# Two-branch attention with a routed mixture of experts on one core: the order of copies, scores and weighted sums within a head pair, and the engine of expert 0's low halves

## What is computed

```python
# attention, for each batch and head: the sum of two branches
q_d, k_d, v_d = means over 4 neighbouring tokens          # 144 rows
out_d = softmax(scale * q_d @ k_d.T) @ v_d                # downsampled branch
out_up = repeat(out_d, 4)
scores = where(|i - j| < 4, scale * q @ k.T, -1e9)        # local branch
x = out_up + softmax(scores) @ v                          # 2304 tokens x 512
# dense layer
h = x @ w_in; x2 = (h * cos(h)) @ w_out                   # 512 -> 2048 -> 512
# experts: each token goes to the one of 8 with the largest logit
e = argmax(x2 @ w_gate); g = softmax(x2 @ w_gate)[e]
out = g * (relu(x2 @ w1[e]) @ w2[e])                      # 512 -> 1024 -> 512
```

## Time and profile before

| | us |
|---|---|
| median of 3 executions | 1009.35 |
| lowest and highest | 1007.31 and 1009.55 |
| the profiled execution | 1010.8 |
| its span | 1009.1 |
| TensorE busy in it | 879.5 (87%) |
| VectorE busy | 563.1 (56%) |
| ScalarE busy | 388.0 (38%) |
| GpSimd busy | 340.0 (34%) |

### The profile page before, as it was taken

How to read it: one execution, slowest core, us unless ns; L and a number is a source line. 1 busy time by engine, 2 the same in 40 slices (tenths; PEclk the granted TensorE clock), 3 DMA queues, 4 the chain that set the end, 5 groups by cost and what they waited for, 6 DMA issues and landing times.

```text
span 1009.1 us, 16491 instructions
## 1 busy us (share of the span) xinstructions
PE 879.5 (87%) x5833; PEld 747.2 (74%) x5834; DVE 563.1 (56%) x846; ACT 388.0 (38%) x670; POOL 340.0 (34%) x445
## 2 busy tenths in 40 slices
PE   3877778768999999999999999980499999999996
PEld 2665656556788988988989979960388888888885
DVE  1666666657665664665665665639255255255521
ACT  3444443434344343343343343323145245245521
POOL 4655455614333333333332332415111211112221
PEclk9866666769999999999999999985599999999999
DMA  6654554202000000000000002033263364254211
GB/s 151 153 134 127 140 139 106 69 18 91 1 1 32 1 1 31 0 0 31 0 0 31 0 23 92 1 115 104 83 209 123 115 208 138 102 202 152 89 40 39
DMA packets 90557, 77.97 MB, mean 77 GB/s; under 512 B 65550, under 2 KB 70158, under 8 KB 90512
## 3 DMA queue, kind: packets, MB, share of 16 engines
q1 hardware_dynamic: 83504, 57.97, 19.5%
q0 software_dynamic: 3680, 11.02, 3.2%
q10 hardware_dynamic: 3328, 8.39, 2.5%
HBM read 67.91 MB, written 10.49 MB: 78 GB/s over the span
## 4 chain that ended last, share of the span: by engine, by line
PE 71%; DVE 14%; ACT 6%; issue 4%; DMA 1%; SPq 1%; POOL 1%; ACTq 0%; DVEq 0%; POOLq 0%
PE psum L1199 16%; PE psum L1213 15%; PE psum L1293 12%; PE psum L1310 12%; PE psum L1153 2%; DVE angle L914 2%; PE psum L1302 2%; PE psum L1116 2%; PE psum L1228 2%; PE psum L1137 2%; DVE probs L842 1%; ACT probsT L674 1%; DVE max_l L839 1%; DVE angle L911 1%; DVE turns L909 1%
## 5 line engine op out<-in xcount | busy, mean ns | idle before, releaser
L1199 PE MATMUL psum<-x_hi,w_in 128*128 128x384 f32 x768 | 218.5, 345 | 9.8 <-DVE turns L917 8.7
L1213 PE MATMUL psum<-w_out,g_hi 128*128 128x512 f32 x576 | 182.0, 397 | 9.3 <-ACT x L733 6.3
L1199 PEld LDWEIGHTS psum<-x_hi,w_in 128*128 128x128 f32 x768 | 142.4, 190 | 19.7 <-DVE turns L917 13.9
L565 POOL TENSOR_SCALAR g_hi<-turns 128x384 fp32r<-128x384 f32 x96 | 53.5, 558 | 288.5 <-DVE turns L917 286.1
L721 ACT ACTIVATE angle<-angle 128x384 f32<-128x384 f32 x96 | 50.4, 525 | 256.9 <-DVE angle L914 256.9
L1199 PE MATMUL psum<-x_lo,w_in 128*128 128x384 f32 x384 | 130.7, 340 | 0.0
L1213 PEld LDWEIGHTS psum<-w_out,g_hi 128*128 128x128 f32 x576 | 106.3, 188 | 30.6 <-ACT x L733 6.1
L917 DVE TENSOR_TENSOR turns<-angle,psum 128x384 f32<-128x384 f32 x96 | 53.2, 555 | 120.3 <-ACT angle L723 120.3
L1293 PE MATMUL psum<-w,xg_hi 128*128 128x512 f32 x352 | 113.8, 405 | 1.4 <-DVE xg_lo L1032 1.4
L1310 PE MATMUL psum<-w,hT_hi 128*128 128x512 f32 x352 | 114.0, 405 | 0.0
L1213 PE MATMUL psum<-w_out,g_lo 128*128 128x512 f32 x288 | 113.8, 395 | 0.0
(11 more groups left out here) (154 smaller groups left out, 1346.3 us busy)
## 6 DMA issues: line engine op xcount, KB each, us to landing
raw_e<-in_moe_w_dram SPq DMA_DIRECT2D x64, 512.0 KB, 6.1
v_win<-in_v_dram SPq DMA_DIRECT2D x192, 28.0 KB
q_nat<-in_q_dram SPq DMA_DIRECT2D x32, 144.0 KB, 3.1
k_nat<-in_k_dram SPq DMA_DIRECT2D x32, 144.0 KB, 3.2
v_grp<-in_v_dram SPq DMA_DIRECT2D x32, 144.0 KB
x_rows<-x SPq DMA_DIRECT2D x18, 256.0 KB, 2.0
raw<-in_moe_w_in_dram ACTq DMA_DIRECT2D x8, 512.0 KB, 3.7
raw<-in_moe_w_out_dram ACTq DMA_DIRECT2D x8, 512.0 KB, 3.5
```

Source lines behind the costliest of these rows:

```text
L565: pool.tensor_scalar(g_hi[r][:, :], turns[r][:, :], 1.0, 1.0, ALU.mult, ALU.mult).then_inc(ghi_done, 1)
L1199: ins = pe.matmul(ps_h[r][:, 0:BT], w_in[:, a, k, cut], x[:, k, :], start=k == 0 and a == 0 and x is x_hi, stop=k == KC - 1 and a == 1)
L1213: ins = pe.matmul(ps_acc[t][:, :], g[r][:, cut], w_out[:, f, a, :], start=f == 0 and g is g_hi and a == 0, stop=f == FC - 1 and g is g_lo)
```

## The change

1. ScalarE: the two `pT_copy` of pair i come ahead of `exp_local` of pair i+1.
2. VectorE: `shift_down` of pair i+1 comes ahead of `pT_down_copy` of pair i.
3. TensorE: `score_down` of pair i+1 comes ahead of `weigh_local` of pair i.
4. GpSimd makes no low halves for expert 0. VectorE makes all eight: two between the last one-hot column and the wait for the ids, six after the ids.

```diff
--- before.py
+++ after.py
@@ -65,7 +65,6 @@
 PIECES_FF = 2 * KC * FF // PIECE
 PIECES_EARLY = 10
 PIECES_E = 2 * KC * F2 // PIECE
-POOL_PIECES = 5
 
 
 def window_start(b):
@@ -592,12 +591,6 @@
             pool.sem_inc(route_const, 1)
 
 
-            for n in range(POOL_PIECES):
-                pool.wait_ge(ehi_done, n + 1)
-                hi, lo, src = piece_e(0, n)
-                pool.tensor_tensor(lo, src, f32(hi), ALU.subtract).then_inc(elo_done, 1)
-
-
             pool.wait_ge(ids_ready, 1)
             total = pool.value_load(first_tile[0:1, E:E + 1], min_val=E, max_val=MAX_TILES)
             def gather(g, n):
@@ -691,11 +684,11 @@
                 if i + 2 < PAIR_ALL:
                     turn_copy(i + 2, 0)
                     turn_copy(i + 2, 1)
-                if 0 <= i + 1 < PAIR_ALL:
-                    exp_local(i + 1)
                 if i >= 0:
                     pT_copy(i, 0)
                     pT_copy(i, 1)
+                if 0 <= i + 1 < PAIR_ALL:
+                    exp_local(i + 1)
                 if i + 2 < PAIR_ALL:
                     turn_copy(i + 2, 2)
                     turn_copy(i + 2, 3)
@@ -888,10 +881,11 @@
                 if 0 <= i + 1 < PAIR_ALL:
                     shift_local(i + 1)
                     inverse_local(i + 1)
+                if 0 <= i + 1 < PAIR_ALL:
+                    shift_down(i + 1)
                 if i >= 0:
                     pT_down_copy(i)
                 if 0 <= i + 1 < PAIR_ALL:
-                    shift_down(i + 1)
                     inverse_down(i + 1)
                 if i >= 0:
                     combine(i, 0)
@@ -936,6 +930,12 @@
             ff_block(BLOCKS - 1, True)
             for t in range(TT):
                 x2T_copy(TT * (BLOCKS - 1) + t)
+
+
+            def split_e(e, par, n):
+                dve.wait_ge(ehi_done, PIECES_E * e + n + 1)
+                hi, lo, src = piece_e(par, n)
+                dve.tensor_tensor(lo, src, f32(hi), ALU.subtract).then_inc(elo_done, 1)
 
 
             done = [0]
@@ -1005,6 +1005,8 @@
                                      gate_b[:, 2, :].unsqueeze(2).broadcast_to(wide))):
                 dve.tensor_tensor(cols[:, :, c, :], is_a[:, :, :], val, ALU.mult).then_inc(cols_ready, 1)
             dve.tensor_copy(cols[:, :, 5, :], is_a[:, :, :]).then_inc(cols_ready, 1)
+            for n in range(2):
+                split_e(0, 0, n)
             dve.wait_ge(ids_done, 1)
             then(dve.tensor_copy(id_f[:, :, :], ps_id[:, 0:6 * ID_TILES].rearrange("p (c n) -> p c n", c=6)))
             then(dve.scalar_tensor_tensor(out=id_t[:, :], in0=id_f[:, 1, :], scalar=float(P), in1=id_f[:, 0, :],
@@ -1017,14 +1019,7 @@
             then(dve.tensor_tensor(gate_s[:, 0:ID_TILES], gate_t[:, :], id_f[:, 4, :], ALU.add))
             dve.sem_inc(ids_ready, 1)
 
-            def split_e(e, par, n):
-                dve.wait_ge(ehi_done, PIECES_E * e + n + 1)
-                hi, lo, src = piece_e(par, n)
-                dve.tensor_tensor(lo, src, f32(hi), ALU.subtract).then_inc(elo_done, 1)
-
-
-            dve.wait_ge(elo_done, POOL_PIECES)
-            for n in range(POOL_PIECES, PIECES_E):
+            for n in range(2, PIECES_E):
                 split_e(0, 0, n)
 
             def xg_copy(g):
@@ -1178,10 +1173,10 @@
                     turn(i + 2, 3)
                 if i >= 0:
                     probs_turn_down(i)
-                    weigh_local(i)
                 if 0 <= i + 1 < PAIR_ALL:
                     score_down(i + 1)
                 if i >= 0:
+                    weigh_local(i)
                     weigh_down(i)
```

## The result

| | before | after |
|---|---|---|
| median, us | 1008.33 (1005.46 to 1009.55, 4 runs) | 968.21 (966.90 to 969.04, 4 runs) |
| ratio | | 0.9605, 95% interval 0.958 to 0.963 |
| profiled execution, and its span | 1010.8, 1009.1 | 967.9, 966.2 |

The change makes the kernel 40.1 us faster; the forecast was 36.3 us, at 973. Two marks in VectorE's timeline divide the two profiled spans: the start of the copy of the last logits (routing begins) moved from 681.72 to 648.24, and TensorE's first turn of gathered rows from 720.48 to 677.08. So 33.5 us were gained ahead of routing and another 9.9 us in it (38.76 us against 28.84). Behind that first turn nothing was gained (288.6 us to the end of the span before, 289.1 after). These stages add up to 42.9 us, the difference of the two spans.

What follows compares the result with a forecast made beforehand. VectorE's in-order list, stretched by waits, was taken to set attention's period (13.07 us), and VectorE's chain alone the routing. Attention 27.4 plus routing 8.9 gave 36.3 us off 1010.8: 974.5, or 973 for the median; range 958 to 990.

Steps and rivals of the forecast that it cites:

- The exponential's delay: Attention, ScalarE: the copies now ahead of it delay the exponential by some 0.25 us, hidden before VectorE's next need.
- The split periods: Attention: nine periods ending in a pair behind a weight split, from 12.96 to 10.65 us each, 20.8 us gained.
- a: Attention: the forecast's time origin, the start of the local maximum, also the end of the local scores on TensorE.
- The plain periods: Attention: five periods without a weight split, from 11.48 to 10.65 us each, 4.1 us gained.
- The rest of attention: After the last local maximum: the downsampled chain starts 2.2 to 3.4 us earlier, taken as 2.5 us gained.
- Loads: Attention: SyncE's loads of queries, keys and values are for two pairs later, with a period of cover; cost 0.
- rival 4: Attention does not move, bound by loads or another queue; only routing gains: 1000.5 us, chance 0.03.
- The 1 us for six loads instead of three: Routing: three more loads of expert 1 leave beside the first gather; bounds 0 and 3.5 us, cost taken as 1.
- The full clock: Attention: TensorE's clock stays full; periods a+10.0 with a split, 9.0 without; about 958 us, chance 0.15.
- The low clock: Attention: TensorE stays at the low clock; period 11.8 us, 19.9 us gained in all, 989.5 us, chance 0.22.
- The gather that waits for six splits: Routing: the first gather waits for the splits, losing 4.6 us in place of 1; 976.6 us, chance 0.10.
- rival 5: Attention: a circle with GpSimd waiting for whole weight splits takes 14.5 us; 4.4 us slower, 1014 us, chance 0.03.

Runs made afterwards that it cites:

- e3: The changed kernel with ScalarE's copies of the turned probabilities behind the exponential again: 987.34 us, ratio 0.9807 to the kernel before.
- e4: The changed kernel with VectorE's copy of the turned probabilities ahead of the downsampled maximum again: 967.32 us, ratio 0.9598 to the kernel before.
- e12: The changed kernel with downsampled copy on ScalarE, GpSimd's scaling ahead of value sums, and expert 1 loads held until first gathered rows are turned: 960.32 us, ratio 0.9533.
- e5: The changed kernel with TensorE's local weighted sum ahead of the downsampled scores again: 974.39 us, ratio 0.9658 to the kernel before.
- e1: Attention only: edits 1 to 3 of the change, with the routing of the kernel before: 978.32 us, ratio 0.9706 to the kernel before.
- e11: The changed kernel with SyncE's loads of expert 1 held until TensorE has turned the first gathered rows: 966.42 us, ratio 0.9576 to the kernel before.
- e7: The changed kernel with VectorE's six splits held until TensorE has turned the first gathered rows: 972.34 us, one execution.
- e10: The changed kernel with VectorE's weight split moved into its wait for the local exponential: 967.97 us, ratio 0.9607 to the kernel before.
- e8: The changed kernel with the copy of the turned downsampled probabilities moved from VectorE to ScalarE: 965.40 us, ratio 0.9582 to the kernel before.

## Why the prediction was right, and where it was not

**The sign and the size.** 40.1 us gained, 36.3 forecast; the median of 968.2 lies within the range and 4.8 us under the forecast. The terms are compared in the two profiles, where they add up to 43.4 us (33.5 and 9.9) against 36.3. So the sum of the misses below is 7.1 us, and the medians make the forecast look better than its terms were.

**ScalarE's order.** Right, and shown by e3: the wait of 2.90 us for the copy was the cause, worth 19 us. The exponential's delay is hidden, as stated.

**The split periods**, 20.8 us forecast, 22.2 measured. The steps from a = 101.92 in the changed kernel: the downsampled turn at a+2.04 (by the forecast's terms a+2.2), maximum of the downsampled scores at a+3.81 (3.85, set by VectorE as forecast). The copy ends at a+5.95 (6.2). Then the forecast had TensorE back at the low clock, 1.16 for the sum and a+10.65 for the scores. The sum ran at the full clock, 0.71, and the clock fell only at the queries (1.19), so that the scores end at a+9.96. VectorE's side, forecast at 10.4, set the period at 10.35. So the step that put TensorE last (a+10.65, with VectorE's side at 10.4) failed. VectorE's number came out right by luck: its split starts at a+8.39, 0.35 earlier than forecast, and takes 2.04 instead of 1.66, since it waits for the whole of GpSimd's `v_half`. The step that failed there is the split's price, taken from a row of before in which GpSimd's place in its list was another. e4 shows that VectorE's own order does not set that end: in another order its list ends at the same time.

**The plain periods**, 4.1 us forecast, 7.7 measured. I took one number, 10.65, for both kinds. Plain ones took 9.93: no weight split lies in them, and three of the five end with the maximum waiting 1.7 to 1.9 us for TensorE's scores. TensorE ran there at a mean granted clock of 0.84 (0.67 in the plain periods before). That the clock made them shorter is argued, not shown, and what ends the last two is not known. This is the largest miss, 3.6 of the 7.1 us.

**The rest of attention.** From the last maximum to the routing 2.9 us (2.5 forecast; with the same attention code, 2.4 to 3.0 in other profiles); the first period 0.7, which I had left alone. Sum: 22.2 + 7.7 + 2.9 + 0.7 = 33.5.

**Loads.** Costed at 0, and nothing shows a cost. At 10.15 us (e12) SyncE's queue still keeps up; rival 4 is out.

**Edits 2 and 3** were not priced apart from each other. e4 shows 0 for edit 2, and e5 up to 6 us, outside the steady state, for edit 3.

**Routing.** The 9.9 us from the small instructions are right to 0.1. The 1 us for six loads instead of three did not come, as the landing took 7.6 us both times. It scatters, though: with three loads it took 7.6 (before) and 6.9 (e1), with six 7.4 to 8.0 in nine profiles, so three more loads cost less than a microsecond. No row was behind the bound of 3.5 us for them; e11 shows that without any loads the landing is 2.8 us sooner. Whether three loads already fill the gather's way was not tried.

**The rivals.** The full clock was the nearest one by its numbers: 0.81 on average, and the measured time lies between its 958 and the forecast. As a cause it fails for the split periods, since e4 has the same period at a lower clock. The low clock did not come. The gather that waits for six splits is excluded: its issue began at 669.45 and ended at 671.72, in the midst of the splits, which run to 674.00. The splits do lengthen the issue, by 1.0 us (2.27 against 1.25 in e7), which is less than one split. The circle of rival 5, with the slower outcome, exists in another form: GpSimd and VectorE do wait for each other's whole instructions, once in each pair with a split, for some 0.9 us each, on a circle of 10.34 us that is short enough to leave the gain.

## What to carry to other kernels

On engines that run strictly in order, look for the copy that others wait for and that stands behind an instruction with a wait of its own; moving it ahead was about half of this gain (19 of 40 us). When several edits of one engine's list leave the period the same to 0.01 us, look for a circle through another engine: follow the steps on the timeline, end to start, with no wait for anything outside, and then shorten one step to see whether the period follows. An edit that gains nothing alone can gain once a second bound, close behind the first, is moved as well, so test the small ones together. And a time of a single instruction can hold a wait for another engine (1.66 us here for a split that takes 1.2 alone): compare it with the shortest of its kind before it becomes a price.

## What was not expected of the hardware

- A 64-column subtraction on VectorE, with both inputs in SBUF, takes 0.30 us if it begins 0.22 us ahead of the end of GpSimd's instruction, and 1.07 us if it begins 0.99 ahead. The two engines alternate by whole instructions: a split of 1.2 us (e10) takes 2.0, a value sum of 0.73 us takes 1.59, `v_half` 2.25 instead of 1.27.
- TensorE can turn the rows of an indirect gather about 2.5 us after the end of its issue (673.04 to 675.57 in e7), and 5.4 us after it with the loads of 512 KB pieces beside it (671.72 to 677.08).
- The mean granted clock in attention rose from 0.68 to 0.81 with the change, while it was busy for less of the same 140 us (103.9 against 108.1). In e4, with the same steady period, it is 0.69 from 40 to 123 us, against 0.81.
- The steady period (10.33 to 10.36 us in the changed kernel, e1, e4, e7, e8 and e11) repeats closely, but the first pairs and the plain ones do not. With the same attention code, the profiled routing starts were 648.24, 650.19, 650.88 and 651.08 (the changed kernel, e1, e7, e11). A difference of under 3 us in this stage can't be read from one profile.
